# A fused attention and two-MLP kernel: its front stage unrolled and reordered up to unit two

## The reference

```python
qn = q / (norm(q, axis=1) + 1e-6)            # norm over the 6016 rows, per column
kn = k / (norm(k, axis=1) + 1e-6)
s = kn.T @ qn / tau                          # 256 x 256
a = softmax(s, axis=-1)
x = v @ a                                    # 6016 x 256
h = x @ w_in1;  x = (h * sigmoid(1.702 * h)) @ w_out1
h = x @ w_in2;  out = where(h > 0, h, exp(min(h, 0)) - 1) @ w_out2
```

## Time and profile before

| what | us |
|---|---|
| median of three runs | 1059.29 |
| lowest and highest | 1058.21, 1060.09 |
| the profiled execution | 1059.76 |
| its span (first to last instruction) | 1058.0 |
| TensorE busy in the span | 1033.8 (98%) |
| VectorE busy | 771.9 (73%) |
| ScalarE busy | 764.6 (72%) |
| GpSimd busy | 61.8 (6%) |

### The profile page before, as it was taken

The page is one execution under the profiler, slowest core; times in us unless marked ns, Lnnn a source line. Parts: engine busy times, 40 slices in busy tenths (PEclk is TensorE's granted clock), DMA queues, the critical chain, the costliest instruction groups (busy, mean ns, idle before and its releaser), DMA issues.

```text
span 1058.0 us, 14064 instructions
## 1 busy us (share of the span) xinstructions
PE 1033.8 (98%) x4614; PEld 861.4 (81%) x4614; DVE 771.9 (73%) x1206; ACT 764.6 (72%) x1368; POOL 61.8 (6%) x54
## 2 busy tenths in 40 slices
PE   9879999999999999999998999999999999999996
PEld 8768888888888888888897887887888888888896
DVE  8877766655656656555778887888887887788775
ACT  7676766566566656556678888788788788888874
POOL 0042300000000000000333000000000000000000
PEclk9989999999999999999999999999999999999999
DMA  9933003002102102003113001201201110110112
GB/s 316 268 81 60 1 1 75 6 1 60 20 1 60 18 1 58 1 1 120 41 40 115 1 1 43 38 1 41 41 1 40 21 20 17 39 21 1 21 21 36
DMA packets 113528, 46.25 MB, mean 44 GB/s; under 512 B 98992, under 2 KB 104112, under 8 KB 112816
## 3 DMA queue, kind: packets, MB, share of 16 engines
q1 hardware_dynamic: 113456, 45.36, 16.2%
HBM read 33.03 MB, written 12.32 MB: 43 GB/s over the span
## 4 chain that ended last, share of the span: by engine, by line
PE 88%; ACT 5%; issue 3%; DVE 2%; DMA 1%; ACTq 0%; DVEq 0%; SPq 0%
PE bank L933 29%; PE bank L935 28%; PE bank L934 28%; PE bank L946 1%; ACT xo L610 1%; DMA qk<-in_k_dram 1%; ACT act_out L580 1%; ACT blk_hi L479 1%; DVE gated L830 1%; ACT g_hi L598 0%; DVE sumsq L681 0%; PE bank L995 0%; PE bank L996 0%; PE bank L1000 0%; PE bank L940 0%
## 5 line engine op out<-in xcount | busy, mean ns | idle before, releaser
L843 DVE TENSOR_TENSOR g_lo<-gated,g_hi 128x512 fp32r<-128x512 f32 (+1 forms) x384 | 264.3, 689 | 49.6 <-ACT g_hi L598 43.6
L933 PE MATMUL bank<-g_hi,w_dn_hi 128*128 128x512 f32 (+1 forms) x768 | 296.3, 386 | 0.8 <-DVE g_lo L843 0.8
L934 PE MATMUL bank<-g_lo,w_dn_hi 128*128 128x512 f32 (+1 forms) x768 | 295.8, 385 | 0.0
L935 PE MATMUL bank<-g_hi,w_dn_lo 128*128 128x512 f32 (+1 forms) x768 | 295.7, 385 | 0.0
L933 PE MATMUL bank<-blk_hi,w_up_hi 128*128 128x512 f32 (+1 forms) x672 | 262.5, 391 | 8.3 <-DVE h L817 4.0
L934 PE MATMUL bank<-blk_lo,w_up_hi 128*128 128x512 f32 (+1 forms) x672 | 259.4, 386 | 0.0
L935 PE MATMUL bank<-blk_hi,w_up_lo 128*128 128x512 f32 (+1 forms) x672 | 259.4, 386 | 0.0
L598 ACT CAST g_hi<-gated 128x512 fp32r<-128x512 f32 (+1 forms) x288 | 175.6, 610 | 21.7 <-DVE gated L830 21.7
L933 PEld LDWEIGHTS bank<-g_hi,w_dn_hi 128*128 128x128 f32 x768 | 144.2, 188 | 29.0 <-DVE g_lo L843 2.0
L935 PEld LDWEIGHTS bank<-g_hi,w_dn_lo 128*128 128x128 f32 x768 | 144.2, 188 | 26.9
L934 PEld LDWEIGHTS bank<-g_lo,w_dn_hi 128*128 128x128 f32 x768 | 144.2, 188 | 26.8
(11 more groups left out here) (114 smaller groups left out, 803.9 us busy)
## 6 DMA issues: line engine op xcount, KB each, us to landing
qk<-in_q_dram SPq DMA_DIRECT2D x15, 384.0 KB, 3.9
qk<-in_k_dram SPq DMA_DIRECT2D x15, 384.0 KB, 5.4
x_scratch<-xo SPq DMA_DIRECT2D x10, 512.0 KB, 3.1
raw<-x_scratch SPq DMA_DIRECT2D x5, 1024.0 KB, 4.8
out_dram<-blocks SPq DMA_DIRECT2D x40, 128.0 KB, 2.7
blocks<-in_v_dram SPq DMA_DIRECT2D x36, 128.0 KB, 3.2
stage<-in_moe_w_in_dram SPq DMA_DIRECT2D x8, 512.0 KB, 8.1
stage<-in_moe_w_out_dram SPq DMA_DIRECT2D x8, 512.0 KB, 4.9
```

Of the source, the lines that this page charges most:

```text
L843: nc.vector.tensor_tensor(g[1][:, x, 0:w], gated[:, n % 2, 0:w], g[0][:, x, 0:w].bitcast(F32), ALU.subtract).then_inc(c_glo, 1)
L933: nc.tensor.matmul(out_ps, w_hi, x_hi, start=start, stop=False, skip_group_check=goes_on)
L934: nc.tensor.matmul(out_ps, w_hi, x_lo, start=False, stop=False, skip_group_check=goes_on)
L935: return nc.tensor.matmul(out_ps, w_lo, x_hi, start=False, stop=stop, skip_group_check=goes_on)
```

## The change

In the front the loops are written out. There are 17 groups (2 steps, 14 times 3, 2, 1) in a ring of five; 19 steps are split, not 15: one in each of groups 1 to 11, then 2, 1, 2, 2, 1. The low parts are made by GpSimd, not VectorE. Squares are added into three PSUM banks, and folded into `sumsq` while the last groups still run; the squares of the last group go to a bank of their own. The sums over partitions (`norms`) stand on TensorE after the whole steps of group 14 and ahead of the last split steps. `w_in1` is split by ScalarE (high) and GpSimd (low) alone; the loads of v come behind all q and k and three blocks of `w_in1`; the loads of `w_out1` wait until the squares are added, since a buffer of theirs holds squares. Idle matmuls are three turns, not five.

```diff
-    RING = 4
+    SPLIT = 2
+    RING = 5
+    PARTS = 3
+    G_STEPS = [2] + [3] * 14 + [2, 1]
+    G_SPLIT = [0] + [1] * 11 + [2, 1, 2, 2, 1]
+    SQUARES_UP_TO = list(range(1, 12)) + [13, 15, 16, 17, 17, 17]
...
+            sums = early.enter_context(nc.psum_tensor("sums", [P, GROUP, 2, C], F32))
...
 @block.sync
+            for n in range(NG):
+                load_group(n)
+                if n == NG // 2:
+                    sp.dma_start(tau_sb, tau.to_broadcast([P, 1])).then_inc(c_tau, 16)
+            for fb in range(FB - 1):
+                load_w_in1(fb)
+            load_v(blocks, 0, 0, c_v)
+            load_v(first_blocks, 0, 1, c_vsecond)
+            load_w_in1(FB - 1)
+            sp.wait_ge(c_sum, SUM_ZERO + NG - 1)
             for qu in range(2):
                 load_w_out(qu, w_out1, qu)
...
 @block.gpsimd
+            for i, n in enumerate(SPLIT_GROUPS):
+                pool.wait_ge(c_qkhi, i + 1)
+                steps = slice(0, G_SPLIT[n])
+                nc.gpsimd.tensor_tensor(qk_s[1][:, i % PARTS, :, steps, :], qk[:, n % RING, :, steps, :],
+                                        qk_s[0][:, i % PARTS, :, steps, :].bitcast(F32), ALU.subtract).then_inc(c_qklo, 1)
+            for fb in range(FB):
+                pool.wait_ge(c_w1hi, fb + 1)
...
 @block.scalar
+            for n in range(NG):
+                if n in SPLIT_GROUPS:
+                    split_hi(n)
+                while squared < SQUARES_UP_TO[n]:
+                    square(squared)
+                    squared += 1
             w1_hi(0)
...
             nc.scalar.activation(small[:, 1:2], small[:, 1:2], ACT.Exp)
+            w1_hi(1)
             w1_hi(2)
-            w1_hi(3)
...
 @block.vector
+                part = sums[:, 0:G_STEPS[n], :, :].rearrange("p s a c -> p a s c")
+                nc.vector.tensor_tensor(part, part, sq[n % 2][:, :, 0:G_STEPS[n], :], ALU.add).then_inc(c_sum, 1)
...
+            for n in range(NG - 2):
+                add_squares(n)
+            nc.vector.tensor_copy(sumsq[:, :, :], sums[:, GROUP - 1, :, :]).then_inc(c_fold, 1)
+            add_squares(NG - 2)
+            for lane in reversed(range(GROUP - 1)):
+                fold_lane(lane)
+            nc.vector.tensor_tensor(sumsq[:, :, :], sumsq[:, :, :], sq_last[:, :, 0, :], ALU.add).then_inc(c_fold, 1)
...
 @block.tensor
+            for n in range(NG):
+                whole_steps(n)
+                if n == NG - 3:
+                    norms()
+                if n in SPLIT_GROUPS:
+                    split_steps(n)
```

```diff
 ScalarE
+            block_hi(0, X11)
+            nc.scalar.activation(small[:, 1:2], small[:, 1:2], ACT.Gelu_apprx_sigmoid)
+            block_hi(0, X21); aw_raw(0); aw_raw(1); up_hi(0, 0); w1_hi(3); aw_raw(2); up_hi(0, 1)
+            block_hi(0, T2); aw_raw(3); block_hi(0, T1); dn_hi(0); up_hi(0, 2); block_hi(0, T3)
+            copy_u1(0); block_hi(0, T4); aw_raw(4); block_hi(0, X22); up_hi(1, 0); copy_u2(0)
+            aw_raw(5); aw_raw(6); gelu(0, H11); copy_u3(0); g_hi(0, H11); up_hi(1, 1); aw_raw(7)
+            gelu(0, H22); gelu(0, H21); g_hi(0, H22)
 VectorE
+            transpose_v(0, 0); reciprocal(inv_sum); eT_lo; block_lo(0, X11); transpose_v(0, 1)
+            t_of(0, T1); block_lo(0, X21); t_of(0, T2); up_lo(0, 0); t_of(0, T3); up_sums(0)
+            block_lo(0, T2); block_lo(0, T1); up_lo(0, 1); t_of(0, T4); up_lo(0, 2); block_lo(0, T3)
+            block_lo(0, T4); sum11_of(0); up_sums(1); up_lo(1, 0); block_lo(0, X22); sum22_of(0)
+            g_lo(0, H11); dn_lo(0, 0); up_lo(1, 1); dn_lo(0, 1)
 TensorE
-            a_w 0 to 4; product1(0); product2(0); a_w(5); product6(0); product5(0); a_w(6)
-            product7(0); a_w(7); product4(0); product3(0)
+            a_w 0 to 3; product1(0); a_w(4); a_w(5); product2(0); a_w(6); product6(0); product1(1)
+            product7(0); product5(0); a_w(7); product4(0); product2(1); product3(0)
 VectorE, weights(U)
-                    if U == at:
+                    if U == at and U:
+                        up_sums(n)
                         up_lo(n, 0)
                         up_lo(n, 1)
                     if U == at + 1:
                         up_lo(n, 2)
+                        dn_lo(n, 0)
+                        dn_lo(n, 1)
```

More of the change, by code:

```diff
@@ L38, in attention_and_two_mlps @@
     GROUP = 3
-    RING = 4
-    NG = -(-STEPS // GROUP)
-    G_LOOP = NG // RING - 1
+    SPLIT = 2
[4 more added lines that the diff above has]
+    SQUARES_UP_TO = list(range(1, 12)) + [13, 15, 16, 17, 17, 17]
+    NG = len(G_STEPS)
+    G_AT = [sum(G_STEPS[:n]) for n in range(NG)]
+    SPLIT_GROUPS = [n for n in range(NG) if G_SPLIT[n]]
     FB = F // BANK
@@ L666, in unit @@
                 g_hi(U, H22)
-            for U in range(ALL + 1):
+            for U in range(1, ALL + 1):
                 unit(U)
@@ L673, in _ @@
             nc.vector.memset(scores[:, :, :], 0.0).then_inc(c_zero, 1)
-            for half in range(2):
-                nc.vector.memset(sumsq[:, half, :, :], 0.0).then_inc(c_sum, 1)
-            def add_squares(place, steps, turn):
-                dve.wait_ge(c_sq, turn * RING + place + 1)
-                dve.wait_ge(c_sum, turn * RING + place + 2)
-                part = sumsq[:, :, 0:steps, :]
-                nc.vector.tensor_tensor(part, part, sq[:, place % 2, :, 0:steps, :], ALU.add).then_inc(c_sum, 1)
@@ L696, in _, with add_squares @@
-            sums(0)
-            with dve.Fori(1, G_LOOP) as turn:
-                sums(turn)
-            sums(G_LOOP, last_turn=True)
+            for lane in range(GROUP):
+                nc.vector.memset(sums[:, lane, :, :], 0.0).then_inc(c_sum, 1)
+            def add_squares(n):
+                dve.wait_ge(c_sq, n + 1)
+                dve.wait_ge(c_sum, SUM_ZERO + n)
+                part = sums[:, 0:G_STEPS[n], :, :].rearrange("p s a c -> p a s c")
+                nc.vector.tensor_tensor(part, part, sq[n % 2][:, :, 0:G_STEPS[n], :], ALU.add).then_inc(c_sum, 1)
@@ L940, in _, with whole_steps @@
                     nc.tensor.matmul(s_ps[i], scores[:, 0, 0:P], scores[:, 0, :], start=turn == 0, stop=False)
-            def score_group(place, steps, turn, last=False):
-                pe.wait_ge(c_qk[place], turn * 32 + 32)
-                for s in range(0 if last else 1, steps):
+            def whole_steps(n):
+                pe.wait_ge(c_qk[n % RING], 32 * (n // RING + 1))
+                for s in range(G_SPLIT[n], G_STEPS[n]):
                     for i in range(KC):
-                        mm = nc.tensor.matmul(s_ps[i], qk[:, place, 1, s, i * P:(i + 1) * P], qk[:, place, 0, s, :],
-                                              start=False, stop=last and s == steps - 1)
-                if last:
+                        mm = nc.tensor.matmul(s_ps[i], qk[:, n % RING, 1, s, i * P:(i + 1) * P], qk[:, n % RING, 0, s, :],
+                                              start=False, stop=False)
+                if not G_SPLIT[n]:
@@ L949, in score_group @@
                     mm.then_inc(c_score, 1)
-                    return
-                pe.wait_ge(c_qklo, turn * RING + place + 1)
-                hi, lo = (part[:, place % 2, :, :] for part in qk_s)
-                for i in range(KC):
-                    rows = slice(i * P, (i + 1) * P)
-                    mm = three_pass(s_ps[i], hi[:, 1, rows], lo[:, 1, rows], hi[:, 0, :], lo[:, 0, :], False, False)
-                mm.then_inc(c_score, 1)
-            with pe.Fori(0, G_LOOP) as turn:
-                for r in range(RING):
-                    score_group(r, GROUP, turn)
@@ L970, in _, with split_steps @@
-            mm.then_inc(c_norm, 1)
+            def split_steps(n):
+                at = SPLIT_GROUPS.index(n)
+                pe.wait_ge(c_qklo, at + 1)
+                hi, lo = (part[:, at % PARTS, :, :, :] for part in qk_s)
+                for s in range(G_SPLIT[n]):
+                    for i in range(KC):
+                        rows = slice(i * P, (i + 1) * P)
+                        mm = three_pass(s_ps[i], hi[:, 1, s, rows], lo[:, 1, s, rows], hi[:, 0, s, :], lo[:, 0, s, :],
+                                        False, n == NG - 1 and s == G_SPLIT[n] - 1)
+                mm.then_inc(c_score, 1)
@@ L1080, in unit @@
                 product3(U)
-            for n in range(5):
+            for n in range(4):
                 a_w(n)
             product1(0)
+            a_w(4)
+            a_w(5)
             product2(0)
-            a_w(5)
+            a_w(6)
             product6(0)
+            product1(1)
+            product7(0)
             product5(0)
-            a_w(6)
-            product7(0)
             a_w(7)
             product4(0)
+            product2(1)
             product3(0)
```

353 lines of the change are left out of this document (155 added, 198 removed).

## The result

The changed kernel takes 1050.15 us (median of four runs, 1049.37 to 1051.19), the kernel before 1059.69 in runs beside it (1058.21 to 1060.68): a ratio of 0.9912, 95% interval 0.9895 to 0.9929. The forecast was 1050.0. The parts are less near than the sum: in the profiled execution one gained 2.7 us less than forecast and one 2.2 us more.

The account below looks back on a forecast made before the run. TensorE bounds the kernel from 81 us on; the loss lies ahead, in the norms' path, a wait and half clock. 1059.76 - 7.3 - 3.3 + 1.3 = 1050.5 profiled, 1050.0 median; range 1045.5 to 1057.0, the forecast's own 1047.5 to 1052.5.

Parts of the forecast that it names:

- Step 1: Front: the scores end earlier, so VectorE's scaling of them starts at 46.3 instead of 53.59: -7.3 us.
- The scaling, named as a sign: End of the front: VectorE's scaling of the scores starting at 45.5 to 47 would show the forecast right.
- The first three-step group: Start of the front: TensorE waits there for data and the group's low part, 0.5 us.
- Group 14: Late front: its load is issued at 29.4 and lands at 34.8; the squares TensorE awaits for the norms follow.
- the rival that the front is late: End of front: GpSimd's low parts take 1.66, or the root waits for `w_in1`; +3.2 us, 1053.2; chance 0.19.
- Step 2: First `a_w` to first `down`: 21.1 us instead of 24.4, product 3's wait for Gelu's table gone: -3.3 us.
- The wait of product 6: Unit 0: TensorE waits 2.0 us for `up_lo`, late on VectorE, which loses 2.4 beside GpSimd's fourth `w_in1` low part.
- the half-clock stretch that I left at the first `a_w`: Around the first `a_w`: TensorE's first stretch at 1.2 GHz stays, since TensorE still idles before it; 1.7 us.
- the rival "better": TensorE's short rest does not lower the clock and the collision misses the path: -1.7 and -2.0, 1046.3; chance 0.12.
- Step 3: Later units: VectorE takes over 21.5 us of GpSimd's sums and `dn_lo`; cost +1.3 us, between -1.5 and +6.
- The change to the second MLP: Where the second MLP begins: two late `g_lo` of 0.65 make it 0.5 to 2 us longer.
- the rival on the slower side: Units 1 to 7 and 42 to 49: VectorE becomes the bound; at three quarters of 21.5 us, 1064.8; chance 0.07.

Follow-up runs that it names:

- c2_control: The changed kernel unaltered, run again as control on the chip of two later experiments: 1051.22 us, ratio 0.9923 to the kernel before.
- e0_control: The changed kernel unaltered, run again as control on another chip: 1049.19 us, ratio 0.9905 to the kernel before.
- e5: Changed kernel with the first fourteen load groups of three steps, then 2, 2 and 1: 1049.72 us, ratio 0.9904 to the kernel before.
- e3: Changed kernel with the fourth low half of `w_in1` made by VectorE ahead of T3, not by GpSimd: 1049.17 us, ratio 0.9906.
- f2: Changed kernel with the norms' products behind group 14's split steps instead of ahead of them: 1051.70 us, ratio 0.9921.
- e2: Changed kernel with GpSimd taking back sums of quarters (blocks 2 to 7) and low halves of down weights (1 to 7): 1050.31 us, ratio 0.9916.
- e7: Changed kernel without the early load of the Gelu table on ScalarE: 1051.06 us, ratio 0.9925 to the kernel before.
- f1: Changed kernel with the eighth weight product ahead of product 6 of the first unit, not product 4: 1049.46 us, ratio 0.9907.
- f3: Changed kernel with edits of f2, e3 and f1, plus VectorE's sums for unit 2's weights behind the first `dn_lo`: 1051.18 us, ratio 0.9914.
- f5: Changed kernel with the edits of f2, e3 and f1 together, without f3's edit of VectorE's list: 1049.28 us, ratio 0.9894.
- e6: Changed kernel with the running sums of squares in SBUF instead of PSUM: 1065.24 us, ratio 1.0054 to the kernel before.

## Why the prediction was right, step by step

**Step 1 forecast -7.3 and gave -4.6 in the profiled execution, -6.6 and -5.6 in the controls.** The mechanism holds at each link: the norms ahead of the last scores, squares as the wait (2.20 against 1.8), low parts of 512 elements at 1.29 (1.26 forecast), sums in PSUM at 1.77 (1.76), 4.89 from the norms to the scaling (4.6), and the roots ready 0.98 ahead of the last score (0.8). The scaling, named as a sign between 45.5 and 47, came at 48.98, 47.04 and 48.03. The term that was mis-sized is the loads. Of the 2.7 us in the profiled execution, 2.0 had passed when TensorE was through with the whole steps of group 14 (41.9, forecast 39.9); 0.4 is the longer wait for the squares and 0.3 the longer way from the norms to the scaling. "The first three-step group still waits for data and its low part, 0.5 us" was 2.0: that group starts 3.36 behind a two-step group of 1.73, and takes 2.82 in place of 2.44. The bracket puts 1.28 of it down to k; it has 1.84 in c2_control and 0.56 in e0_control. Another 0.6 went at 40.06 for a low part, late because its high part stands on ScalarE behind the square of group 14, which waits for k. Group 14, forecast to be issued at 29.4 and to land at 34.8, was issued at 31.0 and landed at 36.6 in the profiled execution (34.7 in e0_control), by SyncE's issue of its q and ScalarE's square, released by k:

```profile
31.02 0.33 SPq L286 DMA_DIRECT2D qk<-in_q_dram  x1
...
36.66 1.49 ACT L411 ACTIVATE stage<-qk 128x1536 f32<-128x1536 f32 x1 [0.44 <-DMA qk<-in_k_dram]
```

I had taken the rates of the kernel before, whose first group has three steps; with two steps they fell to between 184 and 273 GB/s from 4 to 5 us in the twelve profiles with that group, where the kernel before had 359. e5 shows that the small group is the cause of the slow start, but not that it is the cause of the late front: there the norms start at 43.10 without it. The last loads differ from execution to execution too (36.6 against 35.6 in c2_control), and the time with them. Of the rival that the front is late, the size came (2.7 us) but neither of its two causes: no root waits for `w_in1`, and GpSimd's low parts take the 1.29 that was counted on.

**Step 2 forecast -3.3 and gave -3.1 (24.38 to 21.32).** The wait of product 6, forecast as 2.0 behind T3's collision of 2.4, is 1.87, with T3 at 2.90 in place of 0.69 beside GpSimd's 2.47; e3 takes the collision away and half the wait goes. One term was right only in sum: the half-clock stretch that I left at the first `a_w` is not there; it came behind product 6's wait, at 66.9, and cost 1.5 there (21.32 against 19.77 in e0). So it is in c2 and f2; in e0, e2, e3, e5, e7, f1, f3 and f5 there is none between the first `a_w` and `down`. That is a half of the rival "better", and it decides between 21.3 and 19.3 to 19.8 for the same order of work. `block_lo` X11 was forecast to start 2.3 us after the first `a_w`; it started 0.7 after it and was stretched to 1.30.

**Step 3 forecast +1.3 and gave -0.9: the sign was wrong.** The units do not keep their spacing: units 3 to 9 take 71.70 us instead of 72.20, and nearly all of that is unit 4, which took 10.65 beside GpSimd's operations (10.64 in e2) and takes 10.19 now. The change to the second MLP is not 0.5 to 2 us longer: TensorE is busy 34.23 of 37.00, as before (34.18), and units 41 to 52 take 119.51 instead of 119.87. The step failed where I added 3.1 us per set to a VectorE time that already held the collisions. From 500 to 553 before, VectorE was busy 42.20 us with 63 operations; now 42.06 with 79. Sixteen more operations and no more time: what GpSimd no longer takes from its rows pays for them, and e2 shows the same the other way round. The lower bound that I named, -1.5 with the collisions alone, was the nearer end. For the same reason the rival on the slower side (VectorE as the bound) had no ground: its 94 to 97% were worked out from stretched rows, and VectorE is now busy 79% and 82% of the two stretches.

The sum in the profiled execution is -4.6 - 3.1 - 0.9 = -8.6 against -9.3 forecast; the medians differ by 9.5. So it is luck that the forecast met the median to 0.2 us: it had two errors of opposite sign, 2.7 and -2.2, and the same program's medians differ by 2 us.

## What to carry to other kernels

Work that is moved from GpSimd to VectorE (or back) must not be priced by adding durations to busy time: rows that ran beside the other engine are too long, and shrink when it stops. A PSUM operand for VectorE can be worth more than the operation itself if GpSimd is to work beside it: here 15 us. And in a front where five engines hand over within 10 us, the next wait stands close behind the one removed (squares, then v, then VectorE's list): none of the six further edits there that were meant to gain (e3, e5, f1, f2, f3, f5) moved the median by more than the 2 us by which one program's medians differ.

## What the runs showed of the hardware that was not expected

- A VectorE addition and a GpSimd subtraction with all inputs in SBUF, each alone 1.76 and 1.29 us, take 2.65 and 2.76 side by side (e6), with one of each per 2.75 us; with the addition's sums in PSUM they take 1.77 and 1.29 side by side (the changed kernel).
- The clock can fall after a short rest of TensorE, and the same rest does not always bring it down: after the wait for the squares it fell behind 1.51 us (f1), 1.70 (e7), 2.08 (e5) and 2.19 (e2), and did not behind 1.22 (e3), 1.56 (e0), 1.65 (c2) and 2.20 (the changed kernel). The stretch at half clock behind it lasted 3.4 us in the four and set back what hung on it by 1.5 (6.4 instead of 4.9 from the norms to the scaling).
- The first loads: 184 to 273 GB/s from 4 to 5 us in the twelve profiles whose first group has two steps (2,048 bytes to a partition) and the next three (3,072), 359 and 384 in the two whose groups all have three there. Why is left open.
